# Attention and expert kernel: scores of the last three batches from rounded high and low parts

## The reference

```python
# B, H, S, D = 4, 8, 768, 64; n_sink, window = 4, 128
scores = scale * np.matmul(q, k.transpose(0, 1, 3, 2))
keep = is_sink | in_window                    # in_window: 0 <= query position - key position < window
scores = np.where(keep, scores, -1000000000.0)
scores = scores - np.max(scores, axis=-1, keepdims=True)
a = np.exp(scores)
a = a / (np.sum(a, axis=-1, keepdims=True) + 1e-09)
out = np.matmul(a, v)                         # per batch and head
# x: (3072, 512), the heads side by side
logits = xc @ w_gate                          # of the tokens with x @ w_skip > 0
h = np.maximum(xc[mask] @ w1[e], 0.0)         # one expert e per token
y[mask] = gate_w[mask, None] * (h @ w2[e])
g = np.maximum(x @ w_in, 0.0) ** 2
result = g @ w_out
```

## Time and profile before

| | |
|---|---|
| median of 3 runs | 924.22 us (922.54 to 924.44) |
| the profiled execution's own time | 924.29 us |
| its span, first to last instruction | 922.8 us |
| TensorE busy (matmul) | 899.4 us, 97% |
| VectorE busy | 473.3 us, 51% |
| ScalarE busy | 421.4 us, 46% |
| GpSimd busy | 81.7 us, 9% |

### The profile page before, as it was taken

How to read it: one execution, slowest core, us unless ns; L and a number is a source line. 1 busy time by engine, 2 the same in 40 slices (tenths; PEclk the granted TensorE clock), 3 DMA queues, 4 the chain that set the end, 5 groups by cost and what they waited for, 6 DMA issues and landing times.

```text
span 922.8 us, 16992 instructions
## 1 busy us (share of the span) xinstructions
PE 899.4 (97%) x5152; PEld 730.2 (79%) x5153; DVE 473.3 (51%) x1419; ACT 421.4 (46%) x970; POOL 81.7 (9%) x147
## 2 busy tenths in 40 slices
PE   7999999989999998999999999999999999999998
PEld 5778777757888886878888888888888888888886
DVE  5787899886776667764242224222422342243224
ACT  7888899835666666553132113221312231232123
POOL 3112121223111111100000000000000000000000
PEclk9999999999999999999999999999999999999999
DMA  5556675285667678740003002100400040004001
GB/s 200 170 160 201 225 239 173 71 296 186 240 248 250 245 245 311 242 106 0 1 36 57 1 1 67 24 0 0 91 0 0 0 91 0 0 0 91 0 0 45
DMA packets 87364, 99.52 MB, mean 108 GB/s; under 512 B 56093, under 2 KB 56221, under 8 KB 87312
## 3 DMA queue, kind: packets, MB, share of 16 engines
q1 hardware_dynamic: 81168, 83.34, 28.6%
q0 software_dynamic: 6000, 15.49, 4.9%
q10 hardware_dynamic: 144, 0.07, 0.0%
HBM read 77.72 MB, written 25.56 MB: 112 GB/s over the span
## 4 chain that ended last, share of the span: by engine, by line
PE 91%; issue 2%; ACT 2%; DMA 2%; DVE 2%; ACTq 1%; DVEq 0%; SPq 0%; POOLq 0%
PE bank L1128 28%; PE bank L1114 28%; PE bank L1029 7%; PE bank L1010 7%; PE bank L869 5%; PE bank L924 4%; PE bank L897 4%; PE bank L935 1%; PE bank L1018 1%; PE bank L949 1%; PE bank L917 1%; DMA w_raw<-in_weights 1%; PE bank L1002 1%; ACT prob L667 0%; DVE x_row L1304 0%
## 5 line engine op out<-in xcount | busy, mean ns | idle before, releaser
L1498 DVE TENSOR_TENSOR g<-relu_c 128x512 f32<-128x512 f32 x96 | 66.4, 692 | 340.7 <-ACT relu_c L812 340.7
L812 ACT ACTIVATE relu_c<-bank 128x512 f32<-128x512 f32 x96 | 57.4, 598 | 371.7 <-PE bank L1114 371.7
L1114 PE MATMUL bank<-x_hi,w_lo 128*128 128x512 f32 x384 | 149.5, 389 | 0.7 <-DVE x_lo L1485 0.7
L1128 PE MATMUL bank<-w_hi,g_lo 128*128 128x512 f32 x384 | 150.1, 391 | 0.0
L1128 PE MATMUL bank<-w_hi,g_hi 128*128 128x512 f32 x384 | 149.4, 389 | 0.0
L1128 PE MATMUL bank<-w_lo,g_hi 128*128 128x512 f32 x384 | 149.4, 389 | 0.0
L1114 PE MATMUL bank<-x_lo,w_hi 128*128 128x512 f32 x384 | 149.4, 389 | 0.0
L1114 PE MATMUL bank<-x_hi,w_hi 128*128 128x512 f32 x384 | 149.4, 389 | 0.0
L667 ACT ACTIVATE prob<-score,neg_max 128x264 f32<-128x264 f32 (+1 forms) x192 | 94.0, 496 | 15.2 <-DVE neg_max L1190 15.2
L1457 DVE TENSOR_TENSOR w_lo<-w_raw,w_hi x70 | 82.0, 1221 | 21.2 <-issue 13.3
L1128 PEld LDWEIGHTS bank<-w_hi,g_lo 128*128 128x128 f32 x384 | 72.1, 188 | 17.3 <-DVE g_lo L1505 2.5
(11 more groups left out here) (149 smaller groups left out, 1280.3 us busy)
## 6 DMA issues: line engine op xcount, KB each, us to landing
w_raw<-in_weights SPq DMA_DIRECT2D x80, 512.0 KB, 4.9
k_in<-in_kT SPq DMA_DIRECT2D x24, 264.0 KB
q_in<-in_qT SPq DMA_DIRECT2D x24, 256.0 KB, 3.4
v_in<-in_v SPq DMA_DIRECT2D x24, 256.0 KB
x_rows<-x_row SPq DMA_DIRECT2D x24, 256.0 KB, 3.3
x_row<-x_rows SPq DMA_DIRECT2D x96, 64.0 KB, 2.4
out<-w_raw SPq DMA_DIRECT2D x12, 512.0 KB, 2.9
x_res<-routed POOLq DMA_DIRECT2D x15, 260.0 KB, 3.4
```

What stands on the lines that cost most here:

```text
L1114: ins = eng.matmul(hc_ps[f % 2][:, :], w[f // UNIT][:, f % UNIT, wcols], x[:, c, :], start=(c == 0 and n == 0), stop=(c == DC - 1 and n == 2))
L1128: ins = eng.matmul(yc_ps[s][:, :], gg[:, f % 2, s * P:(s + 1) * P], w[f // UNIT][:, f % UNIT, DM:CH], start=(f == 0 and n == 0), stop=(f = ...
L1498: eng.tensor_tensor(g[:, f % 2, :], relu_c[:, f % 2, :], relu_c[:, f % 2, :], ALU.mult).then_inc(s_cg, 1)
```

## The change

For tiles 6 to 23 (`IN_PARTS = NT`, the last three batches) the scores are three products of rounded parts, low keys x high queries, high keys x low queries and high x high, added up in the same bank (`scores_in_parts`). They stand pair by pair: both heads of a pair for one product, then both for the next. GpSimd makes the parts in its loop of a tile, between the sinks' parts and the scatter: those of the keys of load i+3 (`split_k`) and of the queries of tile i+2 (`split_q`), a rounding copy and a subtraction each, with a wait between. `q_lo` and `k_lo` lie where `q_in` and `k_in` lie; `k_hi` (a ring of 4) and `q_hi` (2 buffers) are new. To make room, `score` has one buffer per head instead of two, so every maximum now waits for the exponential of the same head in the tile before.

```diff
+IN_PARTS = NT
...
+        q_lo = sb("q_lo", [P, 3, PAIRS, P], F32R, big)
+        k_lo = sb("k_lo", [P, RING, PAIRS, KB], F32R, big)
...
-        score = sb("score", [P, 2, H, 2 * KB], F32, big)
+        score = sb("score", [P, H, 2 * KB], F32, big)
+        k_hi = sb("k_hi", [P, RING, PAIRS, KB], F32R, big)
...
+        q_hi = sb("q_hi", [P, 2, PAIRS, P], F32R, big)
...
+            def split_k(n):
+                part = k_in[:, n % RING, :, :]
+                eng.wait_ge(s_k[n % RING], 16 * (n // RING + 1))
+                eng.tensor_copy(k_hi[:, n % RING, :, :], part).then_inc(s_khi, 1)
+                eng.wait_ge(s_khi, n - IN_PARTS + 1)
+                eng.tensor_tensor(k_lo[:, n % RING, :, :], part, k_hi[:, n % RING, :, :].bitcast(F32), ALU.subtract).then_inc(s_klo, 1)
...
+            def split_q(i):
+                part = q_in[:, i % 3, :, :]
+                eng.wait_ge(s_q[i % 3], 16 * (i // 3 + 1))
+                eng.wait_ge(s_score, H * (i - 1))
+                eng.tensor_copy(q_hi[:, i % 2, :, :], part).then_inc(s_qhi, 1)
+                eng.wait_ge(s_qhi, i - IN_PARTS + 1)
+                eng.tensor_tensor(q_lo[:, i % 3, :, :], part, q_hi[:, i % 2, :, :].bitcast(F32), ALU.subtract).then_inc(s_qlo, 1)
...
+                if IN_PARTS <= i + 3 < TILES:
+                    split_k(i + 3)
+                if IN_PARTS <= i + 2 < TILES:
+                    split_q(i + 2)
...
+                if heads[0] == 0:
+                    eng.wait_ge(s_qlo, i - IN_PARTS + 1)
+                    eng.wait_ge(s_klo, max(own_load(i), own_load(i) if is_first(i) else before_load(i)) - IN_PARTS + 1)
+                for pair in range(heads[0] // 2, heads[-1] // 2 + 1):
+                    for k in range(3):
+                        for half in range(2):
+                            n = H * i + 2 * pair + half
+                            if k == 0:
+                                eng.wait_ge(s_max, n - SCORE_BANKS + 1)
...
+                            qq, kk = ((upper[0], lower[1]), (lower[0], upper[1]), upper)[k]
+                            ins = eng.matmul(score_ps[n % SCORE_BANKS][:, 0:width(i)], qq, kk, start=(k == 0), stop=(k == 2))
+                            if k == 2:
+                                ins.then_inc(s_score, 1)
...
-                if h == 0 and i >= 2:
-                    eng.wait_ge(s_exp, H * (i - 1))
+                if i >= 1:
+                    eng.wait_ge(s_exp, n - H + 1)
```

More of the change, by code:

```diff
@@ L103, in build @@
         masks = sb("masks", [P, 5, 2, KB], F32, big)
-        q_in = sb("q_in", [P, 3, PAIRS, P], F32, big)
-        k_in = sb("k_in", [P, RING, PAIRS, KB], F32, big)
+        loaded = ExitStack()
+        q_in = sb("q_in", [P, 3, PAIRS, P], F32, loaded)
+        k_in = sb("k_in", [P, RING, PAIRS, KB], F32, loaded)
+        loaded.close()
+        q_lo = sb("q_lo", [P, 3, PAIRS, P], F32R, big)
+        k_lo = sb("k_lo", [P, RING, PAIRS, KB], F32R, big)
         v_in = sb("v_in", [P, RING, DM], F32, big)
@@ L211, in build @@
         s_vshi, s_vspart, s_pshi = sem("s_vshi"), sem("s_vspart"), sem("s_pshi")
+        s_khi, s_klo, s_qhi, s_qlo = sem("s_khi"), sem("s_klo"), sem("s_qhi"), sem("s_qlo")
         s_lgT, s_lgturned = sem("s_lgT"), sem("s_lgturned")
@@ L666, in exps @@
                         eng.wait_ge(s_psink, i - 1)
-                    eng.activation(prob[:, i % 2, h, 0:width(i)], score[:, i % 2, h, 0:width(i)], ACT.Exp, bias=neg_max[:, i % 2, h:h + 1],
+                    eng.activation(prob[:, i % 2, h, 0:width(i)], score[:, h, 0:width(i)], ACT.Exp, bias=neg_max[:, i % 2, h:h + 1],
                                    scale=-1.0, accum_out=row_sum[:, i % 2, h:h + 1]).then_inc(s_exp, 1)
@@ L853, in _, with scores_in_parts @@
             eng.sem_inc(s_by, 1)
+            def scores_in_parts(i, heads):
+                at = blocks(i)
+                span = slice(at[0], at[-1] + 1, max(at[-1] - at[0], 1))
+                if heads[0] == 0:
[7 more added lines that the diff above has]
+                                eng.wait_ge(s_max, n - SCORE_BANKS + 1)
+                            rows = slice(half * D, half * D + D)
+                            upper = q_hi[rows, i % 2, pair, :], k_hi[rows, span, pair, :]
+                            lower = q_lo[rows, i % 3, pair, :], k_lo[rows, span, pair, :]
+                            qq, kk = ((upper[0], lower[1]), (lower[0], upper[1]), upper)[k]
+                            ins = eng.matmul(score_ps[n % SCORE_BANKS][:, 0:width(i)], qq, kk, start=(k == 0), stop=(k == 2))
+                            if k == 2:
+                                ins.then_inc(s_score, 1)
             def scores(i, heads):
+                if i >= IN_PARTS:
+                    scores_in_parts(i, heads)
+                    return
                 at = blocks(i)
@@ L1184, in maximum @@
                 eng.wait_ge(s_score, n + 1)
-                if h == 0 and i >= 2:
-                    eng.wait_ge(s_exp, H * (i - 1))
+                if i >= 1:
+                    eng.wait_ge(s_exp, n - H + 1)
                 if h == 0:
                     eng.wait_ge(s_mask, MASKS_MADE[mask_kind(i)])
-                eng.tensor_tensor_reduce(score[:, i % 2, h, 0:width(i)], score_ps[n % SCORE_BANKS][:, 0:width(i)],
+                eng.tensor_tensor_reduce(score[:, h, 0:width(i)], score_ps[n % SCORE_BANKS][:, 0:width(i)],
                                          masks[:, mask_kind(i), 0:len(blocks(i)), :].rearrange("p a k -> p (a k)"), -SCALE, 3.0e38,
```

## The result

The changed kernel takes **947.59 us** (median of 4 runs, 946.51 to 949.68) against 924.33 us of the kernel before on the same chip (median of 4, 922.54 to 925.33): a ratio of 1.0252, 95% interval 1.0235 to 1.027. It is slower, for the reason that the prediction chose, and by 9.6 us more than the 938 predicted. The profiled execution's span is 945.9 us against 922.8.

A forecast was written before the change was run, and what follows sets the result against it. TensorE was taken as the bound, with ScalarE leaving 0.19 us in tiles with weight work. On 924.3 us, VectorE's waits net of the products' gain, 0.8 us in 17 tiles, added 13.6: 938 us, range 921 to 950.

The forecast's parts named there:

- The products: Attention scores, tiles 6 to 23: six steps of 0.12 us make a group 0.93, 1.6 us gained in all.
- Rival 3: Score products of two heads do not run side by side: group 1.65 us, 22.8 us more, 947; chance 0.06.
- GpSimd's cost: GpSimd's splits per tile: copies 0.62 and 0.60 us, subtractions 1.09 and 1.06, together 3.7 with gaps; nobody waits.
- rival 2: GpSimd becomes the bound at its upper ends: loop of 11 us a tile, 979 us; chance 0.04.
- The masked maximum's new wait: VectorE's maximum waits for the previous tile's exponential of the same head, due long before: zero cost.
- The meetings: VectorE's slot selection and candidate product, two SBUF operands each, wait for GpSimd's reads: 0.88 and 0.74 us late a tile.
- the shift of the exponentials: Exponentials, and GpSimd with them, move up to 0.5 us forward against the scores: first wait 0.4, net 0.56 a tile.
- What of them reaches the end: From both waits TensorE loses 0.8 us a tile, the middle of 1.04 and 0.56 net: 13.6 us in 17 tiles.
- The room: Slack of 0.34 us between the fourth maximum's end, 110.91, and TensorE asking for its bank, 111.25.
- The saving: TensorE's shorter score groups: 0.24 us gained per wide tile, 0.19 with weight work; 0.56 lost per narrow tile.
- The case chosen: GpSimd's SBUF reads hold up VectorE's two-operand routing steps: 938 us, 928 to 950; chance 0.55.
- The marks of being right: TensorE idle over 1 us before heads 6 and 7; selection and product lengthened beside k_lo or q_lo; tiles some 8.5.

The follow-up runs named there:

- e4_one_score: The kernel before, with one buffer per head for the masked scores and the wait that goes with it, nothing else: 924.23 us, ratio 1.0002.
- e1_low_zero: The changed kernel, with both low parts filled with zeros by GpSimd instead of subtracted, all twelve score products kept: 922.2 us, ratio 0.9982.
- e2_unused: The changed kernel, with GpSimd's copies and subtractions still made but unused, the scores again float32 products: 948.88 us, ratio 1.0264.
- f1_apart: The changed kernel, with GpSimd's splits moved where few VectorE steps meet them, the key subtraction in four pieces: 927.61 us, ratio 1.0038.
- e6_sum_reduced: The changed kernel, with GpSimd's splits behind the scatter and the exponentials' sums plus 1e-9 formed by a reduction over pairs: 940.8 us, ratio 1.0193.

## Why the prediction was right in sign and short in size

**The products: right.** Steps 0.12 apart, 0.93 a group, both heads of a pair side by side. Rival 3, whose sum of 947 is the measured time, falls by that: the number alone would have spoken for it. Free of waits, wide tiles took 7.54, so 0.22 gained where 0.24 and 0.19 were worked out, and the whole change 2.2 us of span where 1.6 were.

**GpSimd's cost: right for the copies, short for the subtractions.** 0.62 and 0.62 against 0.62 and 0.60 (the mean of 0.67 holds two copies that took 1.08, below); 1.31 and 1.28 against 1.09 and 1.06. From 64 elements at 0.315 to 528 at 1.315 the slope is 2.15 ns an element, not twice 0.83. GpSimd did not become the bound (busy for 5.28 of 8.55 and 5.12 of 8.91 in the tiles shown); rival 2 fell.

**The masked maximum's new wait: right**, zero at the end (`e4_one_score`).

**The meetings: right.** Both steps, at both places, held to the end of GpSimd's instruction. Gross, the prediction had 1.62 us a tile, and 0.5 less after the shift of the exponentials; the middle, 1.37, is 23.3 us in 17 tiles. Measured were 22.3.

**What of them reaches the end: the step that failed.** From the waits of a tile the prediction took 0.34 us of room before head 7 and the 0.24 saved, which left 0.8, 13.6 us in all. (1) The room: none of it is left in the end, 17 x 0.34 = 5.8 us. It is 0.14 instead of 0.34, mostly since the bank counts as free 0.50 behind the maximum's start (84.50 to 85.00), its accumulator read included, and not 0.35, and since the fourth maximum starts 0.07 later (2.21 behind the first where no wait comes, 2.14 before); and the restart takes the 0.14 back. (2) The saving was credited in all 17 tiles, 4.1 us, though narrow tiles lose; measured, it is 2.2: 1.9 us. (3) Waits of 22.3 us cost 25.3: 3.0 us. With 1.0 off for the waits themselves, 13.6 + 5.8 + 1.9 + 3.0 - 1.0 = 23.3, against 23.1 measured. As (3) is what was left over, this sum closes whatever the cause; where (3) lies, the tiles tell.

Against `e1_low_zero` a tile of the changed kernel lasts longer by what its fourth maximum is late (tile 9: 1.00 and 1.00; tile 15: 1.59 and 1.60), except at the ends of batches. Most of (3) is tile 12, the first one behind a narrow tile: 2.88 us longer, with the fourth maximum 0.76 late. Busy us by stretch, tiles 12 and 18 of the changed kernel, then tile 12 of `e1_low_zero`, then of `e2_unused`:

```profile
101.41:110.94 9.53, 8.01 (x60) 6.32 (x62) 7.08 (x41) 6.12 (x23) 5.11 (x8) 0.64 0.44 154
...
157.44:166.19 8.75, 6.67 (x60) 5.14 (x62) 8.05 (x42) 6.84 (x25) 3.72 (x7) 0.80 0.30 98
```
```profile
93.52:100.17 6.65, 5.44 (x63) 4.17 (x64) 6.09 (x40) 5.94 (x23) 2.31 (x6) 1.00 0.53 158
```
```profile
104.25:111.74 7.49, 5.75 (x53) 4.02 (x54) 6.85 (x41) 6.12 (x23) 3.14 (x6) 1.00 0.38 118
```

The clock averages 0.64 in tile 12: from 103.5 to 109.5 TensorE was granted 0.50, that is 1.2 instead of 2.4 GHz. In `e2_unused` the fourth maximum of tile 12 stands just as late, 2.95 behind the first, the clock stays at 1.00, and the tile lasts 7.49 instead of 9.53: by this comparison, an estimate, the fall of the clock is worth 2.0 us. Tile 18, with 0.80, lasts 0.5 longer than its fourth maximum is late. Before the clock fell TensorE had stood idle, for 1.65 us up to 102.89 in tile 12, for 2.25 and 0.59 in tile 18; the kernel before and `e1_low_zero`, which wait 1.0 to 1.1 at the longest in these two tiles, keep 1.00. That the idle time made the clock fall was not tested.

What this idle time has more than in `e1_low_zero` goes back to a meeting that the prediction's list lacks: VectorE's subtraction for the sinks' values (`vs_part`), 64 partitions x 512 with two SBUF operands, which comes once a batch. VectorE and GpSimd at the end of the third batch:

```profile
155.25 1.80 DVE L1371 TENSOR_TENSOR vs_part<-vs_in,vs_part 64x512 fp32r<-64x512 f32 x1
```
```profile
155.19 1.31 POOL L591 TENSOR_TENSOR k_lo<-k_in,k_hi 128x528 fp32r<-128x528 f32 x1
156.45 1.08 POOL L598 CAST q_hi<-q_in 128x512 fp32r<-128x512 f32 x1
```

It takes 1.80 there and 1.20 at the end of the second batch, instead of 0.69, so 1.11 and 0.51 more; TensorE's waits in tiles 18 and 12, 2.25 and 1.65 instead of 1.13 and 1.14, are longer by 1.12 and 0.51. These 1.6 us of VectorE's waits are not among the 22.3.

**The chances.** The case chosen, at 0.55, came; 947.6 lies near the top of its own range of 928 to 950. The marks of being right that the prediction named are in the trace: lengthened steps beside `k_lo` and `q_lo`, tiles of some 8.5, TensorE idle behind the fourth maximum. That idle time comes before head 7 alone, and it is over 1 us (1.17 and 1.18) in four of the tiles with weight work; in the others it is 0.38 to 0.96.

## What to carry to other kernels

Before an idle GpSimd is given SBUF work, list the VectorE steps that will lie beside it, also those that come once a batch: each with two SBUF operands, however small, can cost as much as GpSimd's whole instruction. Cut such work into short instructions, or place it beside steps with one operand in PSUM; test the price first by filling instead of computing. And a room of a few tenths before a wait is not to be subtracted from the wait, unless the restart behind it is priced too.

## What the hardware showed that was not expected

- An addition of a constant and a comparison over 8 float32 elements, one such operand in SBUF, were held by GpSimd's reads (1.27 instead of 0.17; 1.04 instead of 0.23), while a reduction in place of the addition (0.16) was not; nor was the choice of one element, in the form with a scalar from SBUF (0.201 to 0.215 us in all tiles of `f1_apart`).
- GpSimd is held in turn: in the changed kernel `vs_part` ran until 157.05, and the query copy that had started at 156.45 took 1.08 us instead of 0.62. In `e6_sum_reduced` a weight subtraction and the query copy that met took 1.12 and 0.94 us instead of 0.68 and 0.61; which held which, the rows don't tell.
